# Slot 0 ahead of the slot table in a token-routed expert layer: its load, its waits and its products

## Time and profile before

| quantity | value |
|---|---|
| median of 3 runs | 1540.14 us (1539.99 to 1545.33) |
| the profiled execution's own time | 1553.64 us |
| its span, first to last instruction | 1551.9 us |
| PE busy | 1458.8 us, 94% |
| DVE, ACT, POOL busy | 474.2, 480.3, 415.6 us |
| mean granted TensorE clock | 0.975 of full |

### The profile page before, as it was taken

The page is one execution under the profiler, slowest core; times in us unless marked ns, Lnnn a source line. Parts: engine busy times, 40 slices in busy tenths (PEclk is TensorE's granted clock), DMA queues, the critical chain, the costliest instruction groups (busy, mean ns, idle before and its releaser), DMA issues.

```text
span 1551.9 us, 24717 instructions
## 1 busy us (share of the span) xinstructions
PE 1458.8 (94%) x8664; PEld 1174.5 (76%) x8665; DVE 474.2 (31%) x808; ACT 480.3 (31%) x973; POOL 415.6 (27%) x278
## 2 busy tenths in 40 slices
PE   6887369999999999998999999999999999999996
PEld 5655258888888888886888888888888888888885
DVE  3777621111111111113523232322323232332322
ACT  5666123333333333332222222222222222222221
POOL 0244678448266557104501010100101010010100
PEclk9899679999999999999999999999999999999998
DMA  9688345234243343212101010100101000000000
GB/s 309 220 264 250 120 147 159 87 108 133 70 141 108 109 122 115 81 48 90 61 14 42 7 41 14 38 10 14 41 8 41 14 34 14 14 27 0 27 1 27
DMA packets 52860, 122.93 MB, mean 79 GB/s; under 512 B 6609, under 2 KB 12753, under 8 KB 52817
## 3 DMA queue, kind: packets, MB, share of 16 engines
q1 hardware_dynamic: 33728, 79.21, 16.8%
q10 hardware_dynamic: 13136, 24.19, 5.1%
q0 software_dynamic: 5952, 18.92, 3.4%
HBM read 90.78 MB, written 31.52 MB: 79 GB/s over the span
## 4 chain that ended last, share of the span: by engine, by line
PE 90%; DVE 3%; issue 3%; DMA 1%; POOL 1%; ACT 1%; another core or an unknown queue 0%; SPq 0%; ACTq 0%; DVEq 0%; POOLq 0%
PE psum L674 18%; PE psum L676 18%; PE psum L675 18%; PE psum L750 8%; PE psum L748 8%; PE psum L749 8%; PE psum L718 2%; PE psum L507 1%; PE psum L683 1%; PE psum L736 1%; PE psum L568 1%; PE psum L547 1%; POOL x_by_expert L418 1%; PE psum L609 1%; PE psum L622 1%
## 5 line engine op out<-in xcount | busy, mean ns | idle before, releaser
L1241 DVE SCALAR_TENSOR_TENSOR s_r_r<-r_relu,s_col 128x512 f32<-128x512 f32 x144 | 116.1, 806 | 450.4 <-ACT r_relu L972 450.4
L482 POOL DMA_INDIRECT out_dram<-out_sb,out_row_of_y x36 | 36.0, 1001 | 747.2 <-ACT out_sb L982 739.0
L674 PE MATMUL psum<-weights_split,gT_hi 128*128 128x512 f32 x576 | 230.8, 401 | 2.3 <-DVE gT_lo L1243 2.2
L972 ACT ACTIVATE r_relu<-psum 128x512 f32<-128x512 f32 x144 | 86.1, 598 | 471.7 <-PE psum L750 456.9
L675 PE MATMUL psum<-weights_split,gT_hi 128*128 128x512 f32 x576 | 227.7, 395 | 0.0
L676 PE MATMUL psum<-weights_split,gT_lo 128*128 128x512 f32 x576 | 227.6, 395 | 0.0
L750 PE MATMUL psum<-yT_hi,weights_split 128*128 128x512 f32 x576 | 227.2, 394 | 0.0
L748 PE MATMUL psum<-yT_hi,weights_split 128*128 128x512 f32 x576 | 226.1, 393 | 0.1
L749 PE MATMUL psum<-yT_lo,weights_split 128*128 128x512 f32 x576 | 225.8, 392 | 0.0
L396 POOL TENSOR_TENSOR weights_split<-weights_raw,one 128x1024 fp32r<-128x1024 f32 x70 | 135.5, 1936 | 253.9 <-PE psum L676 242.7
L398 POOL TENSOR_TENSOR weights_split<-weights_raw,weights_split 128x1024 fp32r<-128x1024 f32 x70 | 170.0, 2428 | 5.5
(11 more groups left out here) (151 smaller groups left out, 1832.4 us busy)
## 6 DMA issues: line engine op xcount, KB each, us to landing
weights_raw<-in_moe_w_dram SPq DMA_DIRECT2D x64, 512.0 KB
x_slot<-x_by_expert ACTq DMA_DIRECT2D x40, 257.0 KB, 2.8
y_sorted<-y_slot ACTq DMA_DIRECT2D x40, 256.5 KB, 3.3
k_sb<-in_k_dram SPq DMA_DIRECT2D x16, 576.0 KB, 6.5
q_sb<-in_q_dram SPq DMA_DIRECT2D x16, 576.0 KB, 7.7
v_sb<-in_v_dram SPq DMA_DIRECT2D x48, 192.0 KB
y_tile<-y_sorted SPq DMA_DIRECT2D x32, 256.5 KB, 2.7
weights_raw<-in_moe_w_in_dram SPq DMA_DIRECT2D x8, 512.0 KB
```

What stands on the lines that cost most here:

```text
L674: nc.tensor.matmul(dst, lhs[0][:, col:col + P], rhs[0], start=first_, stop=False)
L972: nc.scalar.activation(rel[:], ps[:, HFB + par, :], ACT.Relu).then_inc(rel_done, 1)
L1241: nc.vector.scalar_tensor_tensor(sq[par][:], rel[:], s_col[:], rel[:], ALU.mult, ALU.mult).then_inc(sq_done, 1)
```

## The change

Three things are moved.

1. SP, not ACT, loads slot 0, from the fixed row 0. SP does it after chunk 8 and ahead of chunk 9. It waits for `x_sent[0]` and `x_sent[1]` at 192, and for `x_sent[2]` and `x_sent[3]` at a value from a register. DVE computes that value in two small operations in iteration 15, from expert 0's count after six batches: 96 if the count is 256 or more, else 192.
2. ACT rounds chunks 8 and 9 ahead of the waits for the table; `x_hi(0)` and the first `keep_columns` follow. Then it waits for the same register value and for `tables`, and goes on with `load(1)`, `relu(0)`, `h_hi(0)`, `x_hi(1)`, `load(2)`. DVE runs `x_lo(0)` ahead of the slot table, and after the table `h_lo(0)`, `x_lo(1)`, then `round_low(8)` and `round_low(9)`.
3. PE begins `slot_in(0)` and `slot_up(0)` without waiting for `tables`, with fixed numbers for the weights of slot 0. The order is then `slot_turn(0)`, `slot_in(1)`, `slot_down(0)`, the wait for `tables`, `slot_up(1)`, `slot_in(2)`, `slot_turn(1)`, and the loop from slot 2.

```diff
@@ sync
             for n in (EARLY - 1, EARLY):
                 chunk(n % NCH, n, expert_chunk(n // NCH, n % NCH))
+            sp.wait_ge(need_done, 1)
+            sent = sp.value_load(sent_need[0:1, 0:1], min_val=BATCH_DMA, max_val=2 * BATCH_DMA)
+            for b in range(XBUFS):
+                sp.wait_ge(x_sent[b], 2 * BATCH_DMA if b < 2 else sent)
+            sp.wait_ge(t0_full, UNITS)
+            sp.wait_ge(t1_full, UNITS)
+            sp.dma_start(xin[:], rows_dram[0:P, :]).then_inc(xin_in, 16)
             for n in range(EARLY + 1, 2 * NCH):
@@ tensor
             ranks(B - 1)
             pe.wait_ge(xa_done, UNITS)
-            pe.wait_ge(rank_read, B + 1)
-            pe.wait_ge(tables, 1)
...
-            before3 = pe.value_load(...)
             slot_in(0)
             slot_up(0)
+            pe.wait_ge(rank_read, B + 1)
+            slot_turn(0)
             slot_in(1)
-            slot_turn(0)
-            with pe.Fori(1, before3 + 2) as s:
+            slot_down(0)
+            pe.wait_ge(tables, 1)
+            before3 = pe.value_load(...)
+            slot_up(1)
+            slot_in(2)
+            slot_turn(1)
+            with pe.Fori(2, before3 + 2) as s:
@@ scalar
-            act.wait_ge(tables, 1)
-            before3 = act.value_load(...)
-            for sent in x_sent:
-                act.wait_ge(sent, BATCH_DMA * B // XBUFS)
-            load(0)
+            act.wait_ge(x_sent[0], 2 * BATCH_DMA)
             round_high(EARLY)
             round_high(EARLY + 1)
             x_hi(0)
             keep_columns(0, 0)
+            act.wait_ge(need_done, 1)
+            sent = act.value_load(sent_need[0:1, 0:1], ...)
+            for b in range(XBUFS):
+                act.wait_ge(x_sent[b], 2 * BATCH_DMA if b < 2 else sent)
+            act.wait_ge(tables, 1)
+            before3 = act.value_load(...)
             load(1)
             relu(0)
+            h_hi(0)
             x_hi(1)
             keep_columns(1, 1)
+            for sent in x_sent:
+                act.wait_ge(sent, 2 * BATCH_DMA)
             load(2)
-            h_hi(0)
@@ vector
+                if it == UNITS - 1:
+                    dve.wait_ge(rank_read, B - 1)
+                    nc.vector.tensor_scalar(few_first[:], base[0:1, 0:1], float(2 * P), float(BATCH_DMA), ALU.is_lt, ALU.mult).then_inc(few_done, 1)
...
+                if it == UNITS - 1:
+                    dve.wait_ge(few_done, 1)
+                    nc.vector.tensor_scalar_add(sent_need[:], few_first[:], float(BATCH_DMA)).then_inc(need_done, 1)
...
             positions(B - 1)
+            x_lo(0)
...
-            round_low(EARLY)
-            round_low(EARLY + 1)
             dve.wait_ge(tables, 1)
             before3 = dve.value_load(...)
-            x_lo(0)
-            x_lo(1)
             h_lo(0)
+            x_lo(1)
+            for sent in x_sent:
+                dve.wait_ge(sent, 2 * BATCH_DMA)
+            round_low(EARLY)
+            round_low(EARLY + 1)
```

More of the change, by code:

```diff
@@ L147, in build @@
         x_at = sb("slot_row", [1, SLOTS], I32)
+        few_first = sb("expert_0_is_short", [1, 1])
+        sent_need = sb("sent_before_slot_1", [1, 1], I32)
         starts = sb("slot_starts", [1, E + 1], I32)
@@ L236, in build @@
         tables = sem("tables")
+        few_done, need_done = sem("few_done"), sem("need_done")
         xin_in = sem("xin_in")
@@ L686, in slot_up @@
             def slot_up(s):
-                ready = pe.value_load(w_need[0:1, bass.ds(s, 1)], min_val=KD, max_val=E * NCH)
-                buf = pe.value_load(w_off[0:1, bass.ds(s, 1)], min_val=0, max_val=WBUF)
+                ready, buf = KD, 0
+                if not isinstance(s, int) or s > 0:
+                    ready = pe.value_load(w_need[0:1, bass.ds(s, 1)], min_val=KD, max_val=E * NCH)
+                    buf = pe.value_load(w_off[0:1, bass.ds(s, 1)], min_val=0, max_val=WBUF)
                 pe.wait_ge(conv, ready)
@@ L1157, in _, with round_low, x_lo, h_lo @@
             positions(B - 1)
+            def round_low(n):
+                dve.wait_ge(hi_done, n + 1)
+                dve.wait_ge(conv, n)
+                at = n // NCH * WBUF
+                nc.vector.tensor_tensor(part(at, 1, n % NCH * CH, CH), raw[n % 2][:], part(at, 0, n % NCH * CH, CH), ALU.subtract).then_inc(conv, 1)
+            def x_lo(s):
+                dve.wait_ge(xhi_done, s + 1)
+                nc.vector.tensor_tensor(xT[1][:], ps[:, TXB, :], xT[0][:], ALU.subtract).then_inc(xlo_done, 1)
+            def h_lo(s):
+                for n in range(2):
+                    cols = slice(n * 512, (n + 1) * 512)
+                    dve.wait_ge(hhi_done, 2 * s + n + 1)
+                    nc.vector.tensor_tensor(hT[1][:, cols], ps[:, THB + n, :], hT[0][:, cols], ALU.subtract).then_inc(hlo_done, 1)
+            x_lo(0)
             done = [0]
@@ L1205, in _ @@
             nc.vector.tensor_tensor(y_at[:], x_f[:], x3[:, 2, :], ALU.subtract).then_inc(tables, 1)
[L1207 to L1211, removed]
+            dve.wait_ge(tables, 1)
+            before3 = dve.value_load(slots_m3[0:1, 0:1], min_val=N // P - 3, max_val=SLOTS - 3)
+            h_lo(0)
+            x_lo(1)
+            for sent in x_sent:
+                dve.wait_ge(sent, 2 * BATCH_DMA)
             round_low(EARLY)
             round_low(EARLY + 1)
[L1215 to L1226, removed]
-            x_lo(0)
-            x_lo(1)
-            h_lo(0)
             with dve.Fori(1, before3 + 2) as s:
```

5 lines of the change are left out of this document (3 added, 2 removed).

## The result

The changed kernel takes 1563.85 us (median of 4 runs, 1560.22 to 1565.84) against 1541.79 us for the kernel before (4 runs). The ratio is 1.0132, 95% interval 1.0112 to 1.0152. Measured again later, it was 1.0114 (1.0098 to 1.0130). So it is slower by 18 to 20 us. The direction and the place were forecast; the size was not: 15.3 us and a range that ended at 1560.

The account below looks back on a forecast made before the run. PE was taken to bound the kernel, with a 14.5 us hole at attention's boundary. Delayed table and weights move slot_down(1) from 235.83 to 251.1: 1540.14 + 15.3 = 1555.4 us, own range 1552 to 1559, stated range 1549 to 1560.

Parts of the forecast that it names:

- the hole: PE has nothing to do for 14.5 us between attention's last ranks (end 188.99) and 203.55; the change works on it.
- expert 0's one slot: Expert 0 has one slot, at most 128 rows, so the register gets 192 and slot 1 is expert 1's.
- The short wait: Loading slot 0 after six batches needs 256 rows of expert 0; forecast not to apply, all eight batches awaited.
- rival A: Faster: slot 0 loaded after batch 5, near 183.5, filling PE's idle time; 12.4 us less, 1528 us; 3 in 100.
- Steps 2 and 3: SP issues slot 0's load at 200.25, chunk 9 behind it; slot_up(0) starts at 207.25, 1.0 us late.
- Steps 4 and 5: Slot table on DVE ends at 213.6, its 6.5 us uncovered; ACT issues load(1) at 215.0, before at 206.08.
- Step 6: Weights: round_low(8) and round_low(9) end at 222.4, everything behind moves by 17.6 us; POOL starts chunk 10 at 224.7.
- Step 7: PE: slot_up(1) waits until 233.5 after a hole of 8.7 us; slot_down(1) starts at 251.1 instead of 235.83.
- the same work: Past slot_down(1), slots 0 to 2 up and slot 0 down are done in both; the 15.3 us carries to the end.
- step 1: DVE's two new operations on one number in iteration 15: 0.15 us for both, from 0 to 0.4.
- rival C: Slower still: PE's clock doesn't come back within slot_up(1), 4.6 us in slot_up(2); 1559.5 us; 9 in 100.
- a slow load of slot 1: Rows of slot 1 land 1.9 us late, as the slowest of the 40 loads; in the shift's upper end of 19.

Follow-up runs that it names:

- e1: Changed kernel with DVE's rounding of chunks 8 and 9 moved right behind the slot table, ahead of h_lo(0) and x_lo(1); 1.0089 of the kernel before.
- e3: Changed kernel with DVE's whole order of before (table, both roundings, x_lo(0), h_lo(0), x_lo(1)), SP, ACT and PE as changed; 1.0049 of the kernel before.
- e9: Kernel before with two unused one-number tensors added ahead of the slot starts, moving later operands 64 bytes; 1.0008 of the kernel before.
- e10: Changed kernel with its two new numbers packed into unused bytes of existing tensors, so later addresses are those of before; 1.0106 of the kernel before.

## Why the prediction was wrong in size

- What bounds, the hole, expert 0's one slot: right. The short wait didn't apply, slot 1 belonged to expert 1, and rival A's mark (a load near 183.5) is absent.
- Steps 2 and 3: right. SP's load at L + 3.5 (forecast 200.25 - 196.35 = 3.9), `slot_up(0)` at L + 9.9 (forecast 10.9).
- Steps 4 and 5: right within 1.5 us. Table end at L + 16.0 (17.2), `load(1)` at L + 17.4 (18.6).
- Step 6: right. Chunk 10 on POOL at L + 27.8, forecast 28.3. e1 and e3 show that the late roundings are what holds it, and PE behind it.
- Step 7: right. PE waited 9.48 us (forecast 8.7) and lost its clock; `slot_down(1)` at L + 54.0, forecast 54.75. The boundary costs 14.7 us where 15.3 were forecast.
- Wrong: "Past it, both kernels have done the same work [...] so the shift is carried to the end". Two terms stand behind the boundary that the sum put at nothing. The first: step 1 priced the two new numbers as two operations on DVE. Their cost was the 64 bytes that their tensors take, 3.3 us in the dense stage, shown by e9 and e10. The second: 2.2 us in the last slot's round, where ACT pauses between two issues and PE loses its clock. It is still there in e10 (17.9 us against 16.0), so it doesn't hang on the addresses; its cause is argued above, not tested.
- The parts against the whole: 14.7 at the boundary, 3.3 and 2.2 behind it, less 0.4 in the slots, are 19.8 us, and the traces have 20.2 from L to the last output. The first measurement of the changed kernel gives 0.0132 x 1541.8 = 20.3 us (17.3 to 23.4), the second 0.0114 x 1557.7 = 17.8 us (15.3 to 20.2). The expectation written for the second named 1.0135 or above as the sign of a third part of 2 us; the ratio stayed below, and its interval only just reaches what the traces show.
- The upper end of the range was put at the clock (rival C) and a slow load of slot 1. The 1541.8 us of the kernel before and 19.8 are 1561.6, outside it; the boundary alone would have been inside.
- Rival C's sum has a slip that changes nothing here: 24 products at 0.43 instead of 0.23 us are 4.8 us and not 4.6.

## What to carry to other kernels

A step that is moved forward takes its place in the queue of its engine: list what else on that engine now waits for it, and look above all at the head of a long chain that runs just under the bound. Here two roundings of 2.5 us together, put behind the table and slot 1's rows, cost most of 14.7 us (e3, with them back ahead of both, has 12.8 of it back), while the load that was to be hidden could not move at all on this data. Compare the addresses of all operands before and after any edit that adds a tensor, and try a few offsets of 64 or 128 bytes as an experiment of their own. And when stages behind a change have "the same work", measure them all the same, from an event at the end of the stage that was changed: two of this kernel's three losses stood there.

## What the runs showed of the hardware

The place of its operands in SBUF changes TensorE's pace, with no wait to be seen. With the operands at their old place a dense group takes 90.73 us and a slot 12.51; 64 bytes on, 91.10 and 12.50; 128 bytes on, 90.81 and 12.34; 256 bytes on, 90.73 and 12.51 again. The slot's gain is 1.4% of its time, spread over its products, and PE has no idle time between them. The mean time from the start of a product to the start of the next, from PE's records in the traces (group 2, and six rounds of the slot loop), in ns:

| product (operand that moved) | old place | 64 bytes | 128 bytes | 256 bytes |
|---|---|---|---|---|
| dense, w_in (`yT`, 512 wide) | 229.9 | 233.0 | 233.2 | 229.9 |
| dense, w_out (`gT`, 128x128) | 233.2 | 233.0 | 230.6 | 233.2 |
| slot, w1 (`xT`, 128x128) | 233.3 | 232.4 | 229.3 | 233.3 |
| slot, w2 (`hT`, 128x128) | 233.3 | 233.3 | 229.6 | 233.3 |

In each of these products the other operand, the weights, did not move. By these numbers the place of either kind of operand counts, the 128x128 one too. Against what it counts is open, and so are the addresses between these steps.
